# A fused attention and mixer kernel: the way its weights are split into halves, who splits them, and when they are loaded

## The reference, cut to what matters

```python
# q, k, v: (4, 8, 576, 64).  Attention, twice, and the sum of both:
#  over rows pooled by 4 (144 x 144), and over a band |i - j| < 4
x = (repeat(sm_attn(pool4(q), pool4(k), pool4(v)), 4) + local_attn(q, k, v))   # -> (4, 576, 512)
u = x + real(fft(fft(x, axis=1), axis=2))
un = (u - mean(u)) / sqrt(var(u) + 1e-6)
y = u + maximum(un @ w_ch1, 0) @ w_ch2            # w_ch1 (512, 2048), w_ch2 (2048, 512)
gate = sigmoid(causal_conv5(y, conv_w))
out = (gate * (y @ w_val)) @ w_out
```

## Time and profile before

| | |
|---|---|
| median of 3 runs | 819.88 us (818.84 to 823.23) |
| the profiled execution | 816.47 us, span of its instructions 814.7 us |
| TensorE busy | 728.4 us (89%), granted clock 0.964 over the span |
| VectorE, ScalarE, GpSimd busy | 436.8, 204.7, 65.3 us |
| moved | 49.15 MB |

### The profile page before, as it was taken

How to read it: one execution, slowest core, us unless ns; L and a number is a source line. 1 busy time by engine, 2 the same in 40 slices (tenths; PEclk the granted TensorE clock), 3 DMA queues, 4 the chain that set the end, 5 groups by cost and what they waited for, 6 DMA issues and landing times.

```text
span 814.7 us, 15570 instructions
## 1 busy us (share of the span) xinstructions
PE 728.4 (89%) x5956; PEld 542.8 (67%) x5956; DVE 436.8 (54%) x955; ACT 204.7 (25%) x409; POOL 65.3 (8%) x82
## 2 busy tenths in 40 slices
PE   1838546799999998999999998999999999999998
PEld 1624225577776776787776776777776777777776
DVE  6838769744453585644553584643643681113552
ACT  1206585222221122222221122222211122111101
POOL 3000213000110210000100210000100210000000
PEclk9999555999999999999999999999999999999999
DMA  9991031702200103602200204513100000000001
GB/s 285 285 254 46 2 130 54 170 9 71 62 1 1 59 30 105 127 12 75 48 1 1 59 30 131 104 29 79 26 2 1 0 30 30 2 1 1 1 15 45
DMA packets 42106, 49.15 MB, mean 60 GB/s; under 512 B 4784, under 2 KB 35568, under 8 KB 40944
## 3 DMA queue, kind: packets, MB, share of 16 engines
q1 hardware_dynamic: 33392, 31.69, 16.1%
q10 hardware_dynamic: 8640, 16.43, 6.2%
HBM read 43.38 MB, written 4.72 MB: 59 GB/s over the span
## 4 chain that ended last, share of the span: by engine, by line
PE 72%; DVE 11%; DMA 6%; issue 6%; ACT 3%; POOL 1%; SPq 1%; ACTq 0%; DVEq 0%; POOLq 0%
PE P L499 21%; PE Y L515 21%; PE P L622 4%; PE Y L611 4%; PE Y L622 3%; PE A L524 3%; DMA kl<-qk_win 2%; PE A L486 2%; DMA shared<-v_pool 2%; PE A L479 2%; PE A L469 2%; PE A L411 1%; PE A L572 1%; PE A L422 1%; PE A L566 1%
## 5 line engine op out<-in xcount | busy, mean ns | idle before, releaser
L499 PE MATMUL P<-unT,w 128*128 128x288 f16 x1536 | 210.0, 287 | 8.7 <-issue 4.8
L515 PE MATMUL Y<-hT,w 128*128 128x288 f16 x1536 | 214.9, 286 | 1.5 <-DVE xT L1068 1.5
L1047 DVE SCALAR_TENSOR_TENSOR hT<-P,hT 128x288 f16<-128x288 f32 x128 | 58.3, 456 | 259.1 <-ACT hT L728 259.1
L499 PEld LDWEIGHTS P<-unT,w 128*128 128x128 f16 x1536 | 148.4, 98 | 52.4 <-issue 12.2
L515 PEld LDWEIGHTS Y<-hT,w 128*128 128x128 f16 x1536 | 144.8, 98 | 45.6 <-issue 7.0
L728 ACT ACTIVATE hT<-P 128x288 f16<-128x288 f32 x128 | 52.5, 410 | 193.5 <-PE P L499 193.4
L1083 DVE SCALAR_TENSOR_TENSOR gate<-xT,cw,gate 128x288 f32<-128x288 f32 x128 | 66.4, 519 | 4.5
L699 ACT ACTIVATE prob_or_un<-prob_or_un 73x288 f32<-73x288 f32 (+1 forms) x52 | 23.3, 449 | 141.4 <-DVE prob_or_un L918 141.4
L524 PE MATMUL A<-sdft,pair_or_folded 128*128 128x289 f32 (+5 forms) x102 | 32.7, 443 | 8.7 <-DVE pair_or_folded L975 8.7
L622 PE MATMUL P<-shared,wo 128*128 128x288 f32 x128 | 32.1, 409 | 0.7 <-DVE shared L1095 0.5
L622 PE MATMUL Y<-shared,wo 128*128 128x288 f32 x128 | 32.1, 409 | 0.5 <-DVE shared L1095 0.5
(11 more groups left out here) (147 smaller groups left out, 831.4 us busy)
## 6 DMA issues: line engine op xcount, KB each, us to landing
w<-w_ch ACTq DMA_DIRECT2D x8, 1024.0 KB, 12.0
kl<-qk_win SPq DMA_DIRECT2D x40, 140.0 KB, 5.2
ql<-qk_win SPq DMA_DIRECT2D x20, 256.0 KB, 4.9
vl<-v_win SPq DMA_DIRECT2D x72, 65.0 KB
pair_or_folded<-qk_pool SPq DMA_DIRECT2D x8, 580.0 KB, 4.9
pair_or_spectrum<-qk_pool SPq DMA_DIRECT2D x8, 580.0 KB, 5.3
out<-ot ACTq DMA_DIRECT2D x32, 144.0 KB, 1.8
x<-v_pool SPq DMA_DIRECT2D x4, 576.0 KB
```

Source lines behind the costliest of these rows:

```text
L499: last = mm(P[s % 2][:, 0:HN], w1s[:, k, f * 128:(f + 1) * 128, wt], unT[:, ut, k, ha * HN:(ha + 1) * HN], start=k == 0 and wt + ut == 0, ...
L515: last = mm(Y[d][:, 0:HN], w2s[:, f, d * 128:(d + 1) * 128, wt], hT[s % 3][:, ht, :], start=f == 0 and wt + ht == 0, stop=f == KF - 1 and ...
L1047: nc.vector.scalar_tensor_tensor(out=hT[s % 3][:, 1, :], in0=P[s % 2][:, 0:HN], scalar=0.0, in1=hT[s % 3][:, 0, :], op0=ALU.max, op1=ALU.s ...
```

## The change

- **Place.** w1 gets ten places of 128 x 1024 instead of eight, and is loaded two places up. The split of a chunk goes two places down, high halves packed in one half of the place and low halves in the other. w2 keeps its places, also packed. w_val is now loaded over the last two places of w1, once all of w1 is split.
- **Scale.** The scale comes from the sum of squares: `weight_square` on ScalarE, one chunk in each of the slots 4 to 11, `weight_sum` on TensorE (a product with ones, which takes the place of `partition_all_reduce`), then a chain of small VectorE operations. `weight_max` and `weight_top` are gone.
- **Who splits.** w1: ScalarE writes every high half to its place (no copy back), VectorE makes the low halves of the even chunks, GpSimd those of the odd ones in two operations. w2: GpSimd alone does all eight chunks, in four operations each, after its last `inv_std` of the opening. TensorE waits for them piece by piece: for 1, 2, 4 and 8 chunks at `mlp_down` of slots 0, 2, 4 and 8.
- **Keys.** A third buffer for keys in the opening, over the raw v (`shared`).
- **v.** GpSimd, not VectorE, pools v of element 0 (`first_values`). A small addition is put ahead of GpSimd's memsets.
- **Loads.** w1 in ScalarE's slots 1 to 4; the tables and all of w2 in slots 13 to 15. The first transposes wait for the identity alone, not for all constants.

```diff
-HID_BITS, W2_BITS = 5, 13
+HID_BITS, W2_BITS = 10, 14
...
-        w1 = sb("w1", [128, KD, F])
+        w1_wv = sb("w1_wv", [128, WCH + 2, WCW])
         w2 = sb("w2", [128, KF, DM])
...
+        ql_first = shared[:, 0:4 * 128].rearrange("p (i c) -> p i c", i=4)
+        kl_first = shared[:, 4 * 128:4 * 128 + 16 * WK].rearrange("p (i j c) -> p i j c", i=4, j=2)
...
-        POOLING_FIRST = {1: [("qk", 1)], 2: [("v", 0)], 3: [("v", 1), ("qk", 2)], 5: [("qk", 3)]}
-        WEIGHT_LOADS = [2, 3, 4, 5, 6, 7, 9, 10, 8]
+        POOLING_FIRST = {1: [("qk", 1)], 3: [("qk", 2)], 5: [("qk", 3)]}
+        WEIGHT_LOADS = {1: [0], 2: [1], 3: [2], 4: [3], 13: [8, 4], 14: [5, 6], 15: [7]}
+        SQUARES = {4: 0, 5: 1, 6: 2, 7: 3, 8: 4, 9: 5, 10: 6, 11: 7}
+        W1_HIGH = {12: [0, 1], 13: [2], 14: [3], 15: [4], 16: [5]}
+        W1_LOW = {13: 0, 14: 2, 15: 4}
+        W2_NEEDED = {0: 1, 2: 2, 4: 4, 8: 8}
...
+                    if opening(b) and t == 2:
+                        sp.wait_ge(zeroed, 7)
...
                     pe.wait_ge(hid_sb, n + 1)
+                    if s in W2_NEEDED:
+                        pe.wait_ge(w2_split, W2_NEEDED[s])
                     if s == 0:
-                        pe.wait_ge(w_split, 2 * WCH)
...
+            def weight_sum(i):
+
+                pe.wait_ge(w_squares, WCH * (i + 1))
+                mm((A[0], P[0])[i][:, 0:WCH], one.to_broadcast([128, 128]), wsum[:, i, :], start=True, stop=True).then_inc(w_all, 1)
...
                     for s in range(NU + LAG_T):
+                        if s == W1_AT:
+                            weight_sum(0)
...
                     for j in range(3):
                         mix_feat(b, j)
+                        if j == 0:
+                            weight_sum(1)
...
+                    if c == 2 * KD + 1:
+                        for done in w1_split:
+                            act.wait_ge(done, WCH // 2)
...
             def weight_high(c):
...
+                if c == 0:
+                    act.wait_ge(w_scale, 1)
                 if c >= 2:
-                    weight_in_place(c - 2)
...
+                    act.wait_ge(w1_split[c % 2], c // 2)
+                nc.scalar.activation(wchunk(c, 0), wchunk(c), ACT.Copy, scale=wscale[:, 0:1]).then_inc(w_high, 1)
+
+            def weight_square(c):
+
+                if c % 2 == 0:
+                    act.wait_ge(ld_w[c // 2], 16)
+                if c > 0:
+                    act.wait_ge(w_squares, c)
+                nc.scalar.activation(gate[:].rearrange("p d c -> p (d c)")[:, 0:WCW], wchunk(c), ACT.Square,
+                                     accum_out=wsum[:, c // WCH, c % WCH:c % WCH + 1]).then_inc(w_squares, 1)
...
-                    for c in range(WCH, WCH + 4):
-                        weights(c)
+                    for c in range(WCH, WCH + 2):
+                        weight_square(c)
                     for g in range(5):
                         spectrum(b, g)
+                    for c in range(WCH + 2, 2 * WCH):
+                        weight_square(c)
+                    for c in range(6, WCH):
+                        weight_high(c)
+                    load_weights(2 * KD + 2)
                     for j in range(3):
-                        weights(WCH + 4 + j)
                         odd_part(b, j)
+                    load_weights(2 * KD + 1)
...
                 nc.vector.memset(xT[:, :, 0:TAPS - 1], 0.0)
-                    for c in range(WCH, WCH + 5):
-                        weight_low(c)
+                    weight_low(6)
                     combine(b, 0)
-                    weight_low(WCH + 5)
+                    weight_scale(1)
                     statistics(b, 0)
...
                     if t in FOLD_AFTER:
                         fold_even(b, FOLD_AFTER.index(t))
+                        if first:
+                            weight_low(2 * t - 1)
...
+                if first:
+                    pool.wait_ge(w_scale, 2)
+                    for c in range(WCH):
+                        second_weights(c)
+
+            def first_values(k):
+
+                half = vraw[k].rearrange("p (h r) c -> p h r c", h=2)
+                pool.wait_ge(ld_vraw[k], 16)
+                pt(half[:, 0], half[:, 0], half[:, 1], ALU.add).then_inc(v_half, 1)
+                pool.wait_ge(v_half, k + 1)
+                pt(vd[:, k, :, 0:D], half[:, 0, 0].rearrange("p (h c) -> p h c", h=H), half[:, 0, 1].rearrange("p (h c) -> p h c", h=H),
+                   ALU.add).then_inc(v_pooled, 1)
+
+            def weight_low(c):
+
+                if c == 1:
+                    pool.wait_ge(w_scale, 1)
+                pool.wait_ge(w_high, c + 1)
+                nc.gpsimd.tensor_scalar(wchunk(c), wchunk(c), wscale[:, 0:1], None, ALU.mult).then_inc(w_scaled, 1)
+                pool.wait_ge(w_scaled, c // 2 + 1)
+                pt(wchunk(c, 1), wchunk(c), wchunk(c, 0), ALU.subtract).then_inc(w1_split[1], 1)
+
+            def second_weights(c):
+
+                w, high = wchunk(WCH + c), wtmp[:, c % 2, :]
+                nc.gpsimd.tensor_scalar(w, w, wscale[:, 1:2], None, ALU.mult).then_inc(w_scaled, 1)
+                pool.wait_ge(w_scaled, WCH // 2 + c + 1)
+                nc.gpsimd.tensor_copy(high, w).then_inc(w2_high, 1)
+                pool.wait_ge(w2_high, c + 1)
+                pt(wchunk(WCH + c, 1), w, high, ALU.subtract).then_inc(w2_low, 1)
+                pool.wait_ge(w2_low, c + 1)
+                nc.gpsimd.tensor_copy(wchunk(WCH + c, 0), high).then_inc(w2_split, 1)
...
-            nc.gpsimd.memset(mhalf[:], -0.5).then_inc(init, 1)
+            nc.gpsimd.memset(mhalf[:], -0.25).then_inc(quartered, 1)
+            pool.wait_ge(quartered, 1)
+            pt(mhalf[:], mhalf[:], mhalf[:], ALU.add).then_inc(quartered, 1)
+            nc.gpsimd.memset(mv[:], 1.0).then_inc(init, 1)
             for v in [v[:] for v in vl] + vl_first:
                 nc.gpsimd.memset(v, 0.0).then_inc(zeroed, 1)
             nc.gpsimd.memset(spread[:], 0.0).then_inc(spread_made, 1)
-            pool.wait_ge(ld_const, CONSTS)
+            first_values(0)
+            first_values(1)
+            pool.wait_ge(v_pooled, 2)
+            nc.gpsimd.memset(kl_first, 0.0).then_inc(zeroed, 1)
+            pool.wait_ge(ld_id, 16)
```

More of the change, by code:

```diff
@@ L257, in values, with keys @@
             return vl[t % 2][:], ld_v[t % 2], used if opening(b) else b * (3 - t % 2) + t // 2
+        def keys(b, t):
+            if opening(b) and t == 2:
+                return ql_first, kl_first, ld_qk_first, 1
+            i = (0, 1, 0, 0, 1)[t] if opening(b) else t % 2
+            if opening(b):
+                return ql[i][:], kl[i][:], ld_qk[i], (1, 1, 1, 2, 2)[t]
+            return ql[i][:], kl[i][:], ld_qk[i], b * (3 - i) + t // 2 + i
         def unit_at(b, m, s, lag):
@@ L325, in attend_loads @@
                 load_pair(b, 1)
+                if opening(b):
+                    sp.dma_start(id_sb[:], ident).then_inc(ld_id, 16)
                 load_v(b, 0)
-                if not later(b):
+                if opening(b):
                     load_v(b, 1)
-                    sp.dma_start(id_sb[:], ident).then_inc(ld_const, 16)
                     sp.dma_start(idb_sb[:], identb).then_inc(ld_const, 16)
@@ L346, in attend_loads @@
                 window(b, 1, "v")
-                if not later(b):
+                window(b, 2, "qk")
+                if opening(b):
                     window(b, 2, "v")
-                window(b, 2, "qk")
-                window(b, 3, "qk")
-                if not later(b):
                     window(b, 3, "v")
+                    window(b, 3, "qk")
                     window(b, 4, "qk")
@@ L363, in window @@
                 done = b * NU + UD + t - 1 if t >= 2 else b * NU
-                if what == "v" and opening(b):
-                    done = UD + 1 if t == 4 else 0
+                if opening(b):
+                    done = (UD + 1 if t == 4 else 0) if what == "v" else (0, 0, 0, UD + 1, UD + 2)[t]
                 if later(done):
@@ L413, in unit_scores @@
                     t = u - UD
-                    pe.wait_ge(ld_qk[t % 2], 48 * (b * (3 - t % 2) + t // 2 + 1))
+                    if opening(b) and t == 0:
+                        pe.wait_ge(ld_const, CONSTS)
+                    QL, KL, landed, count = keys(b, t)
+                    pe.wait_ge(landed, 48 * count)
                     mm(S[:, 0:H * LK], idb_sb[:], mask_sb[:, t:t + 1, :].to_broadcast([128, H, LK]),
@@ L421, in unit_scores @@
                             c = WK * (w // 2) + 32 * (w % 2)
-                            last = mm(S4[LQ * w:LQ * w + LQ, half, first:first + 2, :], ql[t % 2][:, i, LQ * w:LQ * w + LQ],
-                                      kl[t % 2][:, i, :, c:c + LK], start=False, stop=True, skip_group_check=True)
+                            last = mm(S4[LQ * w:LQ * w + LQ, half, first:first + 2, :], QL[:, i, LQ * w:LQ * w + LQ],
```

(12 more changed lines are left out.)

158 lines of the change are left out of this document (69 added, 89 removed).

## The result

| | before | after |
|---|---|---|
| median of 20 runs each | 820.88 us (816.98 to 824.29) | 816.47 us (813.89 to 821.4) |
| ratio | | 0.9948, 95% interval 0.9931 to 0.9964 |
| profiled execution | 816.47 us, span 814.7 us | 816.48 us, span 814.6 us |

The account below looks back on a forecast made before the run. TensorE bounds the steady part; gains come from the opening before the first expert product. 19.9 + 1.2 - 2.6 = 18.5, less 2 for handovers: 16.5, so 803.4 us; range 799 to 808, with fast and slow-pass cases 795 to 815.

Parts of the forecast that it names:

- three signs of being wrong in the main: Wait before the ninth down step over 8 us, first product after 128, or a split's scaling on GpSimd over 1.5 us.
- Steady part: After the opening: bound by TensorE, twelve products every 1.47 us; the packed layout of split halves costed at 0.
- Start: Opening until the first value product: GpSimd pools v behind its memsets, first value product at 23.4, 2.8 later than before.
- a price of first use, paid after the change at 0.8 us: GpSimd's first addition: 7.26 us idle, moved from 78.3 to the tiny addition at the start.
- The eighth value product: Global units in the opening: seven units at 3.2 us make 22.4, eighth value product at 45.8, 1.4 late.
- Fourth unit's keys: Local units in the opening: SP's serial issues from 22.5 on, fourth keys landing near 54.
- Scale at 59, third x tile at 66, last x row at 72: End of the local units: w1's scale at about 59, last x row at 72 instead of 84.0.
- One GpSimd split ahead (3.7 us: a scaling of about 1.1 and a subtraction of 2.5), and one between folds. Second fold 76.2: Folds in the opening: third x tile at 66, then GpSimd splits ahead and between, second fold at 76.2.
- From the second fold to the first product: Spectrum until normalisation: products end at 86.5, mix_rev done at 103.5, first product at 120.3, 19.9 earlier.
- Stall: TensorE at down step 8 waits for GpSimd's eight w2 chunks, 6.5 us each: 2.6 us.
- My rival with 7.5 a chunk: GpSimd's passes near 1.5 us: w2 ready at 56, stall 10.6, gain 8.5, 811 us; chance 0.2.
- Transfers and SP decide: Fourth unit's keys land only near 60, local units end at 80, 8 of the gain gone: 812 to 818; chance 0.08.

Follow-up runs that it names:

- a_keys: Changed kernel with only SyncE's issue order changed, keys of the fourth and fifth local units ahead of values of the third and fourth: 810.74 us, ratio 0.9858.
- a_low_dve: Changed kernel with all eight low halves of w1 made by VectorE and none by GpSimd: 810.03 us, ratio 0.9877.
- a_reduce: Changed kernel plus one GpSimd partition_all_reduce whose result nobody uses, ahead of the copy to spread: 816.8 us, ratio 0.997.

## Why the prediction was wrong

Two of my three signs of being wrong in the main came true: the first product after 128 (131.04) and a scaling on GpSimd over 1.5 us (2.84).

- **Steady part: right.** A group of twelve products still starts every 1.47 us; packed halves give nothing and cost nothing.
- **Start: two errors that cancelled.** The first value product came at 20.11, not 23.4. The step "a price of first use, paid after the change at 0.8 us" failed: the addition took 0.20. I had taken the rule of the Trainium skill (GPSIMD Engine Reference, Instruction dispatch) on newly loaded code as one on the first use of an operation, and had not looked for the loading itself. What I booked as the removal of that idle time did go, since the all-reduce went; one addition in the kernel before gives 6.7 us of medians, where the whole change gives 4.4. The eighth value product at 45.13, forecast 45.8, is luck: the seven units took 25.0 us, not 22.4, with 2.60 us of waiting for VectorE's pooling of the second raw pair of q and k (27.25), and 1.93 more behind it.
- **Fourth unit's keys: off by 4.** They landed at 58.0, not 54: the v windows began to be issued at 25.86 and took 13.35 (22.5 and 12.4 forecast, by the earlier trace rows). Price shown by `a_keys`: 2.6 to 3.0 us.
- **Scale at 59, third x tile at 66, last x row at 72: the step that failed first.** They came at 64.8, 72.6 and 80.8. So the path of the local units was 6.6 us late where the folds begin. Besides the keys, and the row of products ahead of the sum, ScalarE's copies to x stood behind a first pass that waited 2.03 us for a low half of VectorE, and one of VectorE's small operations, `lz` at 70.88, took 1.60 us beside GpSimd's split where it takes 0.17 alone.
- **"One GpSimd split ahead (3.7 us: a scaling of about 1.1 and a subtraction of 2.5), and one between folds. Second fold 76.2": mis-sized, and with two terms at nothing.** The second fold ended at 86.1. Of the 9.9 us, 6.6 are the late x tile. The split between the folds took 6.7 instead of 3.7 (3.0 more), but the one ahead lay in waiting time and cost nothing (3.7 less). What the sum had left out without a reason is VectorE's part of the fold behind GpSimd's addition (2.6; 2.25 in the kernel before, by the earlier trace rows) and GpSimd's two memsets and hand-overs ahead of the first addition (1.3). I had priced a scaling by a per-partition number by the copy's row; the copy did take 1.04, so the copy was right and the likeness wrong: the scaling took 2.86 to 3.53. The estimate of about 1.5 us from the figure of the Trainium skill (GPSIMD Engine Reference, Elementwise) would have been too low too. In all, `a_low_dve` puts 5.4 us on GpSimd's splits, less than the 11.5 that the forecast had charged for them (twice 3.7, and 4.1 ahead of `mix_rev`).
- **From the second fold to the first product: right, plus 0.8.** 44.1 us by my steps (76.2 to 120.3), 44.9 measured (86.1 to 131.04). That six squares stood in this chain I had priced; that they need not I had not seen, and it is the largest single reserve (9.0 us).
- **Stall: right place, size off.** Forecast 2.6, measured 4.15: a chunk took 7.24 us, not 6.5, eight were ready 51.9 us behind the first product. My rival with 7.5 a chunk had the ninth step wait 10.6; it waited less, since the batch began 6.1 us ahead of the first product (124.93), not 4, and the need came 47.9 behind it, not 45.4, slots 0 and 1 being slowed by the clock.
- **What I left out.** The clock. A slot product at the lower level costs 1.4 us more; first product to first down step took 11.6 us, 1.7 more than in the profiled execution of the kernel before, and 0.2 to 1.1 more than in its two variants with a tiny addition. Behind the stall another 1.65 went.

In the sum: 19.9 forecast for the start, 9.1 measured; 1.7 of clock not forecast; between the first and the ninth down step 1.4 lost by forecast (2.6 less 1.2), 3.7 measured; 1.65 of clock behind it. That leaves 2.05 us in the profiled execution. Of the rivals, "Transfers and SP decide" (812 to 818) has the time and the end of the local units (80, measured 80.8), but the keys were only 3 us of it. The range failed because all its ends used the same opening up to the second fold.

What stays open: of the 4.4 us of medians and the 2.05 us left at 215 us in the profiled execution, I cannot say which part is the chance of the clock. Why slot 1 ran at full clock in the kernel before and in `a_low_dve`, and wholly or in part at the lower level in the other kernels, no run separates.

## What to carry to other kernels

Price an operation on GpSimd by a row of the same form, not of the same size: a copy, a product with a per-partition number and one of two tensors of 128 x 1024 took 1.04, 2.84 and 1.89 us. When idle time ends with no releaser, look at the sequencer's rows of that line before naming a cause: the same change of code (5.9 to 7.6 us here) was free where nobody waited, and cost all of it behind a late wait. Lay the terms of a forecast beside every engine that a step passes through: VectorE's 2.6 us of each fold were missing here. When an engine issues in order, look for what it could do inside its own wait: moving eight short passes ahead of a wait gained about twice what the whole change did (8.4 us of medians against 4.4).

## What the runs showed of the hardware

- An all-reduce on GpSimd cost 5.9 us ahead of it (`a_reduce`) and 7.1 to 7.6 us ahead of the next arithmetic behind it, each hidden where GpSimd idled between the pair of MODIFY_POOL_CONFIG and the operation; its own time is 0.38.
- GpSimd's product with a per-partition number took 2.84 us for 128 x 1024, more than a product with the same number broadcast as a second tensor (1.89). Beside VectorE the first went to 3.53.
- GpSimd on two tensors holds VectorE off: additions of 255 elements took 2.11 and 2.34 us instead of 0.41. In `a_low_dve` it was the other way round as well: GpSimd's fold took 2.78 beside VectorE's low halves, against 1.26 alone.
- A stall of TensorE of 2.62 to 5.79 us at the ninth down step was followed by twelve products in 2.15 to 3.04 us in six kernels, against 1.64 in the four without a stall: the stall costs more than its own length.
